# Query and key groups of 512 and 256 tokens instead of 384, with expert scores between them

## The chip, the cores and the metric

The kernel runs on one NeuronCore of a Trainium2 chip. The metric is the device time of one execution in microseconds (us); the median of the runs is compared. The engines are called by the profile's names: PE is TensorE (matmuls; PEld are its weight loads), ACT is ScalarE, DVE is VectorE, POOL is GpSimd, SP issues most of the loads and stores. A "wait" is a semaphore wait: each engine runs its own list of instructions in order and stops where a semaphore is not yet high enough.

## What is computed

Three stages, for 4 sequences of 768 tokens with 384 channels. A gated linear recurrence gives x. A mixture of 4 experts, each a causal attention with 64 channels, takes x; a third stage mixes tokens and channels. The change is in the second stage, which per sequence is:

```python
for e in range(E):                       # 4 experts
    q = x @ wq[e]
    k = x @ wk[e]
    v = x @ wv[e]
    scores = scale * (q @ k.transpose(0, 2, 1))
    scores = np.where(causal, -1000000000.0, scores)
    scores = scores - scores.max(-1, keepdims=True)
    a = np.exp(scores)
    a /= a.sum(-1, keepdims=True) + 1e-09
    ye = a @ v @ wo[e]
    # out += (routing weight of e) * ye
```

## The kernel before

The kernel runs the recurrence and the experts for one sequence after the other (`it` is 0 to 3, called the first to the fourth batch here), then the third stage for all four (from about 324 us on). The recurrence of a batch runs on PE with DVE, ACT and POOL preparing the gates of the next batch in whatever gaps they have. The order on each engine is written out by hand; nothing is planned at run time, and only semaphores tie the engines together.

Within a batch the experts start with "ring" groups: PE writes a group into a PSUM bank, counts `ring_done`; ACT rounds it to a high part, counts `ring_hi`; DVE makes the low part (exact minus rounded), counts `ring_free`. A product of two such split operands is three matmuls (L1253, L1254, L1255: high*high, high*low, low*high). The ring has 6 groups that transpose x (`RING_X`), 6 that make the values and gate logits (260 columns each), then the queries and keys: `qk_h`, `qk_l` with four row blocks m = 0 to 3 of 128 rows, 0 and 1 being the queries of experts 0 and 1, and 2 and 3; blocks 2 and 3 the keys of the same pairs. Before the change each block is made in two halves of 384 tokens, so 8 groups of 9 matmuls (3 chunks of channels, 3 products). Group n writes bank n. `qk_of` gives the order: blocks 0, 2 for the first half, 0, 2 for the second, then blocks 1, 3 twice. `FIRST_JOB = 6` puts the scores of the first job behind the sixth of them.

A "job" m (0 to 5) is a pair of query tiles of 128 tokens, (2,3), (1,4) or (0,5), for one pair of experts: `tiles_of(m)` is `TILES[m // 2]` and the expert pair is `m % 2`. So jobs 0 and 1 look at tiles 2 and 3 and need tokens below 512 only; jobs 2 and 3 need tokens up to 640, jobs 4 and 5 all. Job m has 896 score columns per expert in all: the small tile's columns (`which = 0`) at the end of a two-bank tile, the large tile's (`which = 1`) at its start. Both experts of a job fill all of banks 0 to 3. Per job:

- PE, `expert_scores(m)`: the score matmuls L1399 and the mask L1405, in pieces. It waits (`exp_done`) until ACT has read the previous job's scores: for jobs 1 and 2 the first two exponentials are enough for the first pieces, the last one is needed for the last piece; for jobs 3 to 5 all four are needed before any.
- DVE, `row_max(m)`: four reductions L1121, two for each `which`.
- ACT, `exps(m)`: four exponentials L728, each behind its reduction.
- PE, `turn_probs(m, r)`: 14 transposes of 64 columns (L1316) for expert r = 0 or 1, into a pair of banks given by `turn_pair`: banks 4 and 5, but for (0, 1) banks 6 and 7.
- `copy_turned(m)`: ACT copies r = 0 (L769, counts `pt_copied[1]`), DVE r = 1 (L1141, counts `pt_copied[0]`), about 900 columns each.
- PE, `weigh_values(m)`: 28 matmuls L1462.

PE's order around the change is: groups 0 to 5, scores(0), groups 6 and 7, scores(1) (whose last piece waits for all ring groups), turn(0,0), scores(2) with turn(0,1) in it, turn(1,0), weigh(0), turn(1,1), scores(3), and so on. turn(1,0) goes to the banks of turn(0,0) and so waits for ACT's `copy_turned(0)`. DVE's order is: route (a chain of some 25 small operations, L1091 to L1111), low parts of groups 0 to 5 with a prefix scan (L875, 768 columns) for the next batch behind group 3 in the second and third batch, row_max(0), low parts 6 and 7, row_max(1), the first two reductions of row_max(2), copy_turned(0), the other two of row_max(2), `portions(0)` (three small operations), copy_turned(1), row_max(3). ACT's is: groups 0 to 5, exps(0), groups 6 and 7, exps(1), copy_turned(0), first two of exps(2), copy_turned(1), the other two. In the fourth batch ACT also rounds a tile of the token weights (L621) between group 7 and exps(1).

Of the kernel before, what the change touches and what calls it, by code (L numbers as in the profile page):

```python
# [22 lines left out]
P = 128  # L23
B, H, T, HD = 4, 8, 768, 48
D = H * HD
# [113 lines left out]
def turn_pair(m, r):  # L139

    if m == JOBS - 1:
        return r
    return 3 if (m, r) == (0, 1) else 2
# [47 lines left out]
def build(nc, fT, qT, kT, vT, v, wq, wk, wv, w_gate, wo, woT, w_theta, w_tok, w_ch, out):  # L191
    with ExitStack() as ctx:
# [234 lines left out]
        def _(pool):  # L427
# [64 lines left out]
            def token_weights(tile):  # L492

                s, n = tile // 2, tile % 2
# [34 lines left out]
        def _(act):  # L529
# [87 lines left out]
            def token_weights(tile):  # L617

                s, n = tile // 2, tile % 2
                act.wait_ge(tok_in[s], 16)  # L620
                nc.scalar.copy(wt_h[:, n * NT + s, :], wt_raw[:, n * NT + s, :]).then_inc(tok_hi, 1)  # L621
# [43 lines left out]
            for it in range(B):  # L665
# [64 lines left out]

                for n in [*range(RING_X), *range(FIRST_QK, RING)]:
                    if n == FIRST_QK:
# [17 lines left out]
                    if n == FIRST_QK + FIRST_JOB:  # L750
                        exps(0)
                    act.wait_ge(ring_done, upto(it, RING, n + 1))
                    if n < RING_X:
                        nc.scalar.copy(xT_h[:, :, n * P:(n + 1) * P],
                                       ps(ring_bank(it, n))[:, 0:D].rearrange("p (c t) -> p c t", c=NC)).then_inc(ring_hi, 1)
                    else:
                        half, m = qk_of(n - FIRST_QK)
                        nc.scalar.mul(qk_h[:, m, half * HALF:(half + 1) * HALF], ps(ring_bank(it, n))[:, 0:HALF],
                                                                             ED ** -0.5 if m < 2 else 1.0).then_inc(ring_hi, 1)
                    if n == FIRST_QK + 1 and 1 <= it < B - 1:  # L760
                        grow(it + 1, 2)
                    if it < 1 and n == FIRST_QK + 2:
                        shrink_pair(1, 1)
                    if it < 1 and n == FIRST_QK + 3:
                        grow_pair(1, 1)

# [12 lines left out]
                for j in range(JOBS + 2):  # L779
                    if 1 <= j < JOBS:  # L780
# [76 lines left out]
        def _(dve):  # L857
# [143 lines left out]
            for it in range(B):  # L1001
# [122 lines left out]
                for n in range(RING_QK):  # L1124
                    if n == FIRST_JOB:
                        row_max(0)
                        if it < 1:
                            scan(1, 2)
                    dve.wait_ge(ring_hi, upto(it, SPLIT, RING_X + n + 1))
                    half, m = qk_of(n)  # L1130
                    at = slice(half * HALF, (half + 1) * HALF)
                    nc.vector.scalar_tensor_tensor(out=qk_l[:, m, at], in0=ps(ring_bank(it, FIRST_QK + n))[:, 0:HALF],
                                                   scalar=ED ** -0.5 if m < 2 else 1.0,
                                                   in1=qk_h[:, m, at].bitcast(F32), op0=ALU.mult,
                                                   op1=ALU.subtract).then_inc(ring_free, 1)
                    if 1 <= it < B - 1 and n == 3:
                        scan(it + 1, 3)
# [31 lines left out]
                for j in range(JOBS + 2):  # L1169
                    if 1 <= j < JOBS:  # L1170
# [79 lines left out]
        def _(pe):  # L1250
# [61 lines left out]
            for it in range(B):  # L1312
# [69 lines left out]
                def expert_scores(m):  # L1382

                    a = m % 2
                    if m < 1:
                        pe.wait_ge(ring_free, upto(it, RING, FIRST_QK + 4))
                        pe.wait_ge(halves, 128)
                    elif m == 1:
                        pe.wait_ge(ring_free, upto(it, RING, FIRST_QK + 6))
# [25 lines left out]
                    if m == 1:  # L1415
                        pe.wait_ge(ring_free, upto(it, RING, RING))
# [6 lines left out]
                def turn_probs(m, r):  # L1423
# [43 lines left out]
                for n in range(RING):  # L1467
# [9 lines left out]
                    if n == FIRST_QK + FIRST_JOB:  # L1477
                        expert_scores(0)
                    if n < 4:
                        pe.wait_ge(a_masked, upto(it, NT, NT))  # L1480
                    elif n < FIRST_QK and it < B - 1:
# [5 lines left out]
                    elif n < FIRST_QK + 4:  # L1487
                        pe.wait_ge(ring_free, upto(it, RING, n - 3))
                    elif it > B - 2 and n == FIRST_QK + 4:
                        banks_read(0, EARLY)  # L1490
# [7 lines left out]
                    elif n >= FIRST_QK:  # L1498
                        half, m = qk_of(n - FIRST_QK)
                        if n == FIRST_QK:  # L1500
                            pe.wait_ge(wqk_lo, 1)
                        for c in range(NC):
# [134 lines left out]
```

## Time and profile before

| | |
|---|---|
| median of 3 runs | 568.0 us (567.95 to 569.58) |
| the profiled execution's own time | 570.03 us |
| its span, first to last instruction | 568.3 us |
| PE matmuls busy | 538.7 us, 95% of the span |
| DVE, ACT, POOL busy | 371.8, 298.1, 132.0 us (65%, 52%, 23%) |
| TensorE clock granted | 1.000 over the whole span (2.4 GHz) |
| query and key groups start, four batches | 53.91, 127.12, 199.98, 277.37 us |

A busy share of PE counts from the start of a matmul to its modelled end; matmuls overlap, so what a stretch costs is read from start to start. A time written as "+17.65" below is counted from the start of the batch's first query and key group.

### The profile page before, as it was taken

The page shows a single profiled execution, that of the slowest core. Times are in us where ns is not written, and L with a number is a line of the kernel's source. Part 1 is how long each engine was busy: PE and PEld are TensorE (multiplying, and loading weights), DVE is VectorE, ACT ScalarE, POOL GpSimd, SP SyncE. Part 2 cuts the span into 40 slices and gives each one's busy share as a digit, 9 for nine tenths or more (in the row PEclk, how much of TensorE's full clock was granted, in tenths as well). Part 3 has the DMA queues.
Part 4 walks back from the last instruction along what each step waited for, and adds up shares of the span by engine and source line. Part 5 has one row for each costly group of instructions (what it writes and reads, how often), then busy time and mean ns, then how long its engine had stood idle before and what let it go on. Part 6 is the DMA issues. An engine that isn't in the chain of part 4 may idle for free.

```text
span 568.3 us, 14108 instructions
## 1 busy us (share of the span) xinstructions
PE 538.7 (95%) x5996; PEld 508.8 (90%) x5996; DVE 371.8 (65%) x672; ACT 298.1 (52%) x599; POOL 132.0 (23%) x88
## 2 busy tenths in 40 slices
PE   0989999999999999999999999999999999999997
PEld 0688878999789997899978899999999999999997
DVE  2988888878788787775768677555236544462434
ACT  5758687775877548733568664324222433133311
POOL 2003046035510025200022357112211212022200
PEclk9999999999999999999999999999999999999999
DMA  8948013052210430003600000010001100020002
GB/s 289 321 151 301 7 27 86 7 196 112 76 39 3 159 151 2 2 2 104 233 1 2 1 1 2 0 57 29 0 1 43 42 1 1 14 71 1 1 1 83
DMA packets 17969, 37.24 MB, mean 66 GB/s; under 512 B 2160, under 2 KB 10608, under 8 KB 17392
## 3 DMA queue, kind: packets, MB, share of 16 engines
q1 hardware_dynamic: 17904, 36.32, 18.5%
q8 instruction: 47, 0.77, 0.6%
q14 instruction: 18, 0.15, 0.1%
HBM read 31.46 MB, written 4.72 MB: 64 GB/s over the span
## 4 chain that ended last, share of the span: by engine, by line
PE 79%; DVE 8%; ACT 7%; issue 3%; DMA 2%; SPq 1%; DVEq 0%; ACTq 0%
PE bank L1253 18%; PE bank L1254 18%; PE bank L1255 17%; ACT prob L728 5%; PE bank L1462 4%; PE bank L1271 4%; PE bank L1399 4%; PE bank L1316 3%; PE bank L1358 3%; PE bank L1354 2%; DMA OT<-w_theta 2%; PE bank L1339 2%; PE bank L1562 1%; DVE gate L875 1%; DVE nmax L1121 1%
## 5 line engine op out<-in xcount | busy, mean ns | idle before, releaser
L1253 PE MATMUL bank<-z_h,wt_h 128*128 128x384 f32 x288 | 97.7, 339 | 0.0
L1254 PE MATMUL bank<-z_l,wt_h 128*128 128x384 f32 x288 | 97.4, 338 | 0.0
L1255 PE MATMUL bank<-z_h,wt_l 128*128 128x384 f32 x288 | 96.5, 335 | 0.0
L728 ACT ACTIVATE prob<-bank,nmax 128x384 f32<-128x384 f32 (+5 forms) x96 | 60.3, 638 | 20.7 <-DVE nmax L1121 20.7
L524 POOL TENSOR_TENSOR trig<-trig,x 128x768 f32<-128x768 f32 x18 | 33.6, 1865 | 149.6 <-ACT trig L634 92.6
L1121 DVE TENSOR_REDUCE nmax<-bank 128x1 f32<-128x384 f32 (+5 forms) x96 | 54.9, 616 | 10.0 <-PE bank L1405 5.3
L967 DVE TENSOR_SCALAR turns<-bank 128x384 int32<-128x384 f32 x22 | 12.2, 556 | 74.1 <-PE bank L1255 74.1
L1253 PEld LDWEIGHTS bank<-z_h,wt_h 128*128 128x128 f32 x288 | 54.0, 188 | 0.6 <-issue 0.3
L1254 PEld LDWEIGHTS bank<-z_l,wt_h 128*128 128x128 f32 x288 | 54.1, 188 | 0.0
L1255 PEld LDWEIGHTS bank<-z_h,wt_l 128*128 128x128 f32 x288 | 54.0, 188 | 0.0
L843 ACT CAST uT_h<-bank 128x384 fp32r<-128x384 f32 x24 | 11.5, 479 | 78.6 <-PE bank L1562 78.6
L1462 PE MATMUL bank<-probT,Vm 128*64 128x128 f32 x672 | 42.0, 276 | 0.7 <-DVE probT L1141 0.2
L1462 PEld LDWEIGHTS bank<-probT,Vm 128*64 128x64 f32 x672 | 36.2, 137 | 2.9 <-DVE probT L1141 1.4
L626 ACT COPY x<-bank 128x384 f32<-128x384 f32 x24 | 11.6, 481 | 49.8 <-PE bank L1255 44.5
L1007 DVE TENSOR_TENSOR probT<-bank,keep 128x1024 f32<-128x1024 f32 x24 | 29.3, 1221 | 12.0 <-PE bank L1271 11.9
L1358 PE MATMUL bank<-V,probT 128*64 128x48 f32 x768 | 36.1, 219 | 0.4 <-DVE probT L1007 0.3
L1399 PE MATMUL bank<-qk_h 64*128 64x512 f32 (+3 forms) x128 | 26.2, 406 | 7.1 <-ACT prob L728 5.4
L1358 PEld LDWEIGHTS bank<-V,probT 128*64 128x64 f32 x768 | 32.2, 137 | 0.8 <-issue 0.6
L1253 PE MATMUL bank<-xT_h,wqk_h 128*128 128x384 f32 x96 | 32.9, 343 | 0.0
L1254 PE MATMUL bank<-xT_l,wqk_h 128*128 128x384 f32 x96 | 32.4, 337 | 0.0
L1255 PE MATMUL bank<-xT_h,wqk_l 128*128 128x384 f32 x96 | 32.4, 337 | 0.0
L1354 PE MATMUL bank<-S,q 128*64 128x96 f32 x320 | 28.8, 255 | 2.6 <-DVE S L1028 1.9
(177 smaller groups left out, 1398.5 us busy)
## 6 DMA issues: line engine op xcount, KB each, us to landing
V<-v SPq DMA_DIRECT2D x4, 1152.0 KB, 11.1
gate<-fT SPq DMA_DIRECT2D x12, 384.0 KB, 3.2
q<-qT SPq DMA_DIRECT2D x12, 384.0 KB, 6.2
k<-kT SPq DMA_DIRECT2D x12, 384.0 KB, 6.5
wt_raw<-w_tok SPq DMA_DIRECT2D x6, 768.0 KB, 8.5
out<-x SPq DMA_DIRECT2D x24, 192.0 KB, 1.9
gate<-fT SPq DMA_DIRECT2D x3, 512.0 KB, 5.1
q<-qT SPq DMA_DIRECT2D x3, 512.0 KB, 9.5
```

The costliest lines, as they stand in the source:

```text
L524: nc.gpsimd.tensor_tensor(trig[:, s % 2, :, :], trig[:, s % 2, :, :], x2[:, s:s + 1, :].broadcast_to([P, 2, D]), ALU.mult).then_inc(z_made, 1)
L728: nc.scalar.activation(prob[:, m % 2, r, at], bank[r][:, at], ACT.Exp, bias=nmax[:, m, k:k + 1], accum_out=den[:, m // 2, which, e:e + 1]) ...
L1007: nc.vector.tensor_tensor(Am[:, c % 2, :, :], bank[c % 2][:, :].rearrange("p (h t) -> p h t", h=H), keep[:, None, :].broadcast_to([P, H, P ...
L1121: nc.vector.tensor_reduce(nmax[:, m, k:k + 1], bank[r][:, columns_of(m, which)], X, ALU.max, negate=True).then_inc(max_done, 1)
L1253: nc.tensor.matmul(o, a_h, b_h, start=start, stop=False)
L1254: nc.tensor.matmul(o, a_h, b_l, start=False, stop=False)
L1255: return nc.tensor.matmul(o, a_l, b_h, start=False, stop=stop)
L1271: mm = nc.tensor.matmul(bank[c % 2][:, slot(h):slot(h) + P], k[r:r + 64, h // 2, at], q[r:r + 64, h // 2, at], start=True, stop=True)
L1354: nc.tensor.matmul(ps(out_bank(c))[own, h * HD:(h + 2) * HD], q[:, h // 2, c * P + own.start:c * P + own.stop], S[:, c % 2, h // 2, :], st ...
L1358: mm = nc.tensor.matmul(ps(out_bank(c))[own, h * HD:(h + 1) * HD], Am[:, c % 2, slot(h) // P, own], V[:, c, h * HD:(h + 1) * HD], start=(c ...
L1399: mm = nc.tensor.matmul(bank[r][:, lo_:hi_], x[rows, a, queries], y[rows, 2 + a, keys], start=fresh_bank and n == 0, stop=False, skip_grou ...
L1462: mm = nc.tensor.matmul(ps(values_bank(m))[64 * r:64 * r + 64, at], Vm[:, s, e * ED:(e + 1) * ED], probT[:, m % 2, r, n * P:(n + 1) * P], ...
```

## The change

The queries and keys are made in 7 groups: blocks 0, 2, 1, 3 for tokens 0 to 511 (512 columns each), then blocks 0 and 2 for tokens 512 to 767 (256 columns each), then one group with blocks 1 and 3 for tokens 512 to 767 (two of 256 columns in one bank). Groups 0 to 3 come ahead of scores(0), 4 and 5 between scores(0) and scores(1), and the seventh (`LATE_QK = 6`) behind scores(2) and turn(1,0). The number of matmuls and of their columns stays the same, and so does the number of columns on ACT and DVE; the banks, the waits and the orders on DVE and ACT change as the diff shows. In the fourth batch the token weights of a tile pair are taken in the other order.

```diff
-RING_X, RING_QK, RING_V = NT, 8, NT
+RING_X, RING_QK, RING_V = NT, 7, NT
-FIRST_JOB = 6
+FRONT = 4 * P
+LATE_QK = 6
 def qk_of(n):
-    return n % 4 // 2, (0, 2, 1, 3)[2 * (n // 4) + n % 2]
+    if n < 4:
+        return [((0, 2, 1, 3)[n], slice(0, FRONT), slice(0, FRONT))]
+    if n < LATE_QK:
+        return [((0, 2)[n - 4], slice(FRONT, T), slice(0, T - FRONT))]
+    return [(1, slice(FRONT, T), slice(0, T - FRONT)), (3, slice(FRONT, T), slice(T - FRONT, 2 * (T - FRONT)))]
 def ring_bank(it, n):
     if n >= FIRST_QK:
-        return n - FIRST_QK
+        return (0, 1, 6, 7, 4, 5, 6)[n - FIRST_QK]
 def turn_pair(m, r):
-    return 3 if (m, r) == (0, 1) else 2
+    return 3 if (m, r) == (0, 0) else 2
 # POOL and ACT, token_weights
-                s, n = tile // 2, tile % 2
+                s, n = tile // 2, 1 - tile % 2
 # ACT
-                for n in [*range(RING_X), *range(FIRST_QK, RING)]:
+                for n in range(RING_X): ...            # x as before
+                for n in range(LATE_QK):
...
-                    if n == FIRST_QK + FIRST_JOB:
+                    if n == 4:
                         exps(0)
+                    split_qk(n)
...
+                exps(1)
                 for j in range(JOBS + 2):
-                    if 1 <= j < JOBS:
+                    if 2 <= j < JOBS:
                         exps(j, range(0, 2))
-                    if 2 <= j <= JOBS:
+                    if 1 <= j <= JOBS:
                         copy_turned(j - 1)
-                    if 1 <= j < JOBS:
-                        exps(j, range(2, EXPS))
-                    if j == 1:
-                        copy_turned(0)
+                    if 2 <= j < JOBS:
+                        exps(j, range(2, 3))
+                    if j == 2:
+                        split_qk(LATE_QK)
+                    if 2 <= j < JOBS:
+                        exps(j, range(3, EXPS))
 # DVE
+                split_qk(0)
+                split_qk(1)
+                if 1 <= it < B - 1:
+                    scan(it + 1, 3)
+                split_qk(2)
+                if it < 1:
+                    scan(1, 2, 0)
+                split_qk(3)
+                row_max(0)
+                if it < 1:
+                    scan(1, 2, 1)
+                split_qk(4)
+                row_max(1, range(0, 2))
+                split_qk(5)
+                row_max(1, range(2, EXPS))
...
-                    if it < 1 and j == 1:
+                    if it < 1 and j == 2:
                         scan(1, 3, 0)
-                    if j == 1:
-                        row_max(2, range(0, 2))
+                    if j == 2:
+                        split_qk(LATE_QK)
                     if 1 <= j <= JOBS:
                         copy_turned(j - 1)
+                    if j == 1:
+                        row_max(2, range(0, 2))
 # PE, expert_scores
-                    if m < 1:
-                        pe.wait_ge(ring_free, upto(it, RING, FIRST_QK + 4))
+                    if m < 3:
+                        pe.wait_ge(ring_free, upto(it, RING, FIRST_QK + 2 * m + 2))
                         pe.wait_ge(halves, 128)
-                    elif m == 1:
-                        pe.wait_ge(ring_free, upto(it, RING, FIRST_QK + 6))
+                    elif m == 3:
+                        pe.wait_ge(ring_free, upto(it, RING, RING))
...
-                    if m == 1:
-                        pe.wait_ge(ring_free, upto(it, RING, RING))
 # PE, turn_probs
-                    elif m == 1:
-                        pe.wait_ge(pt_copied[1], upto(it, JOBS, 1))
-                    elif m >= 2:
+                    elif m >= 1:
                         pe.wait_ge(pt_copied[0], upto(it, JOBS, m))
 # PE
+                def queries_keys(n):
+                    if n < 2:
+                        pe.wait_ge(ring_free, upto(it, RING, FIRST_V + 2 + n + 1))
+                    elif it > B - 2 and n == 2:
+                        banks_read(0, EARLY)
+                    elif n == LATE_QK:
+                        pe.wait_ge(pt_copied[1], upto(it, JOBS, 1))
...
+                for n in range(4):
+                    queries_keys(n)
+                expert_scores(0)
+                queries_keys(4)
+                queries_keys(5)
+                expert_scores(1)
                 for j in range(1, JOBS + 2):
-                    if j < JOBS:
+                    if 2 <= j < JOBS:
                         expert_scores(j)
...
+                    if j == 2:
+                        queries_keys(LATE_QK)
                     if j >= 2:
                         weigh_values(j - 2)
```

## Rows read from the trace of the kernel before

**Rows 1.** Waits of PE: engine line <- who ended it: us in total, times, longest.

```profile
PE bank L1399 <- ACT prob L728: 5.4, 15, 0.7
```

**Rows 2.** Timeline of PE, third batch: start us, us, engine, line, operation, form, idle before.

```profile
198.03 0.28 PE L1255 MATMUL bank<-wvg_h,xT_l 128*128 128x260 f32 x1
199.98 0.34 PE L1253 MATMUL bank<-xT_h,wqk_h 128*128 128x384 f32 x1
...
209.58 0.44 PE L1399 MATMUL bank<-qk_h 64*128 64x384 f32 x2
...
211.31 0.44 PE L1253 MATMUL bank<-xT_h,wqk_h 128*128 128x384 f32 x1
...
214.66 0.44 PE L1399 MATMUL bank<-qk_h 64*128 64x384 f32 x2
...
217.63 0.39 PE L1399 MATMUL bank<-qk_h 64*128 64x256 f32 x2 [0.20 <-ACT prob L728]
...
218.69 0.60 PE L1316 MATMUL bank<-ident,prob 64*128 64x64 f32 x14
219.26 0.49 PE L1399 MATMUL bank<-qk_h 64*128 64x512 f32 x2
...
220.06 0.65 PE L1316 MATMUL bank<-ident,prob 64*128 64x64 f32 x14
...
223.34 0.39 PE L1399 MATMUL bank<-qk_h 64*128 64x256 f32 x2 [0.30 <-ACT prob L728]
```

**Rows 3.** Timeline of ACT, third batch, the exponentials of jobs 0 and 1.

```profile
211.27 0.58 ACT L728 ACTIVATE prob<-bank,nmax 128x384 f32<-128x384 f32 x1 [1.09 <-DVE nmax L1121]
...
213.72 0.50 ACT L758 ACTIVATE qk_h<-bank 128x384 fp32r<-128x384 f32 x1
...
216.91 0.57 ACT L728 ACTIVATE prob<-bank,nmax 128x384 f32<-128x384 f32 x1
...
218.44 0.68 ACT L728 ACTIVATE prob<-bank,nmax 128x512 f32<-128x512 f32 x1
...
219.10 0.91 ACT L769 COPY probT<-bank 128x896 f32<-128x896 f32 x1
```

**Rows 4.** Timeline of DVE, third batch, low parts, row maxima and the first copy.

```profile
210.21 0.56 DVE L1132 SCALAR_TENSOR_TENSOR qk_l<-bank,qk_h 128x384 fp32r<-128x384 f32 x1 [0.50 <-ACT qk_h L758]
210.69 2.21 DVE L1121 TENSOR_REDUCE nmax<-bank 128x1 f32<-128x384 f32 x4
...
215.76 1.01 DVE L1121 TENSOR_REDUCE nmax<-bank 128x1 f32<-128x384 f32 x2
...
218.90 0.76 DVE L1121 TENSOR_REDUCE nmax<-bank 128x1 f32<-128x256 f32 x2 [0.57 <-PE bank L1405]
219.57 1.08 DVE L1141 COPY probT<-bank 128x896 f32<-128x896 f32 x1
```

**Rows 5.** Timeline of DVE and PE, second batch.

```profile
134.16 1.95 DVE L1132 SCALAR_TENSOR_TENSOR qk_l<-bank,qk_h 128x384 fp32r<-128x384 f32 x4
136.03 1.74 DVE L875 TENSOR_TENSOR_SCAN gate<-fresh,gate 128x768 f32<-128x768 f32 x1
...
138.60 1.00 DVE L1121 TENSOR_REDUCE nmax<-bank 128x1 f32<-128x384 f32 x2
...
127.12 0.34 PE L1253 MATMUL bank<-xT_h,wqk_h 128*128 128x384 f32 x1
...
150.69 0.39 PE L1399 MATMUL bank<-qk_h 64*128 64x256 f32 x2 [0.32 <-ACT prob L728]
```

**Rows 6.** Timeline of PE, first and fourth batch: first group and start of scores(3).

```profile
53.91 0.34 PE L1253 MATMUL bank<-xT_h,wqk_h 128*128 128x384 f32 x1
...
77.28 0.38 PE L1399 MATMUL bank<-qk_h 64*128 64x256 f32 x2
...
277.37 0.34 PE L1253 MATMUL bank<-xT_h,wqk_h 128*128 128x384 f32 x1
...
300.72 0.39 PE L1399 MATMUL bank<-qk_h 64*128 64x256 f32 x2 [0.32 <-ACT prob L728]
```

More of the change, by code:

```diff
@@ L617, in token_weights @@
             def token_weights(tile):
-                s, n = tile // 2, tile % 2
+                s, n = tile // 2, 1 - tile % 2
                 act.wait_ge(tok_in[s], 16)
@@ L729, in exps, with split_qk @@
                                              accum_out=den[:, m // 2, which, e:e + 1]).then_inc(exp_done, 1)
-                for n in [*range(RING_X), *range(FIRST_QK, RING)]:
-                    if n == FIRST_QK:
+                def split_qk(n):
+                    act.wait_ge(ring_done, upto(it, RING, FIRST_QK + n + 1))
+                    for m, tokens, at in qk_of(n):
+                        ins = nc.scalar.mul(qk_h[:, m, tokens], ps(ring_bank(it, FIRST_QK + n))[:, at],
+                                            ED ** -0.5 if m < 2 else 1.0)
+                    ins.then_inc(ring_hi, 1)
+                for n in range(RING_X):
+                    act.wait_ge(ring_done, upto(it, RING, n + 1))
+                    nc.scalar.copy(xT_h[:, :, n * P:(n + 1) * P],
+                                   ps(ring_bank(it, n))[:, 0:D].rearrange("p (c t) -> p c t", c=NC)).then_inc(ring_hi, 1)
+                for n in range(LATE_QK):
+                    if n < 1:
                         if it > B - 2:
@@ L1122, in row_max, with split_qk @@
                                                 negate=True).then_inc(max_done, 1)
[L1124 to L1128, printed above, removed]
-                    dve.wait_ge(ring_hi, upto(it, SPLIT, RING_X + n + 1))
[L1130 to L1137, printed above, removed]
+                def split_qk(n):
+                    dve.wait_ge(ring_hi, upto(it, SPLIT, RING_X + n + 1))
+                    for m, tokens, at in qk_of(n):
+                        ins = nc.vector.scalar_tensor_tensor(out=qk_l[:, m, tokens], in0=ps(ring_bank(it, FIRST_QK + n))[:, at],
+                                                             scalar=ED ** -0.5 if m < 2 else 1.0,
+                                                             in1=qk_h[:, m, tokens].bitcast(F32), op0=ALU.mult,
+                                                             op1=ALU.subtract)
+                    ins.then_inc(ring_free, 1)
+                split_qk(0)
[13 more added lines that the diff above has]
+                row_max(1, range(2, EXPS))
                 def copy_turned(m):
@@ L1169, in _ @@
                 for j in range(JOBS + 2):
-                    if 1 <= j < JOBS:
+                    if 2 <= j < JOBS:
                         row_max(j, range(2 if j == 2 else 0, EXPS))
@@ L1465, in weigh_values @@
                     mm.then_inc(av_done, 1)
-                for n in range(RING):
+                def queries_keys(n):
[5 more added lines that the diff above has]
+                        pe.wait_ge(pt_copied[1], upto(it, JOBS, 1))
+                    if n < 1:
+                        pe.wait_ge(wqk_lo, 1)
+                    for m, tokens, at in qk_of(n):
+                        w = slice(m * P, (m + 1) * P)
+                        for c in range(NC):
+                            mm = split_mm(ps(ring_bank(it, FIRST_QK + n))[:, at], wqk_h[:, c, w], wqk_l[:, c, w],
+                                          xT_h[:, c, tokens], xT_l[:, c, tokens], c == 0, c == NC - 1)
+                    mm.then_inc(ring_done, 1)
+                for n in range(FIRST_QK):
                     if it > B - 2 and n == 0:
@@ L1497, in _ @@
                             mm = nc.tensor.transpose(dst[:, c * P:(c + 1) * P], xn[:, n, c * P:(c + 1) * P], ident[:, :])
[L1498 to L1502, printed above, removed]
-                            at = slice(half * HALF, (half + 1) * HALF)
-                            w = slice(m * P, (m + 1) * P)
-                            mm = split_mm(dst[:, 0:HALF], wqk_h[:, c, w], wqk_l[:, c, w], xT_h[:, c, at],
-                                          xT_l[:, c, at], c == 0, c == NC - 1)
                     else:
```

23 lines of the change are left out of this document (6 added, 17 removed).

## The prediction

> **What bounds the kernel now.** I read the page first (PE 95% busy, full clock), then who PE waits for, then the timelines of PE, ACT and DVE from the first query and key group to the fourth job's scores. All waits of the scores on ACT's exponentials are 5.4 us in 15 places [rows 1]: a mean of 0.36 us. So PE is nearly the bound, and right behind it stands a loop through three engines: scores, row maxima on DVE, exponentials on ACT, next scores. scores(3) starts the moment the last exponential of job 2 is read, after 0.30 us idle, though PE had its other work done [rows 2]. From there on each job hangs on that loop, and it starts from scores(3). So I measure the change by one number: how late scores(3) starts after the batch's first group. Before it is +23.36 in the third batch [rows 2], +23.57 in the second [rows 5], +23.37 and +23.35 in the first and fourth [rows 6]. What moves scores(3) moves the rest of the batch.
>
> **What does not change.** Matmuls of 260 columns go at (199.98 - 198.03)/16 = 0.122 us, of 384 at (209.58 - 199.98 - 0.10)/54 = 0.176, the 0.10 being the switch to another kind [rows 2]. That is 0.436 ns a column, so I take 0.232 for 512 and 0.120 for 256. No row has 512 columns on 128 rows; by proportion it would be 0.235 and not less than the 0.176 of 384. Old: 72 x 0.176 = 12.67 us. New: 36 x 0.232 + 36 x 0.120 = 12.67. Nothing is saved on PE. ACT and DVE have the same columns and eight split operations each as before. The change is one of order.
>
> A rule of the Trainium skill, "TensorE: Matmul & The Clock Gate", section "Back-to-back issue gap", gives N/2.4 + 2.5 ns: 0.216 for 512, 0.1625 for 384, 0.109 for 256. By it the old six groups would take 8.78 us and the new four 7.77, 1.01 earlier instead of the 1.15 below, so 0.14 us a batch worse than my sum. The trace's 384-column gap is 0.176, so it does not agree, and the sum goes by the rows.
>
> **Third batch, step by step** (times from the first group):
> - Groups 0 to 3 end at 36 x 0.232 = +8.35; scores(0) starts at +8.45, before at +9.60 [rows 2].
> - But DVE makes the low part of group 3 ahead of row_max(0). The group is whole at +8.54 (its last matmul 0.23 before the end, and some 0.4 to drain). The split of 384 columns takes ACT 0.50 and DVE 0.56, the next operation starting 0.48 on [rows 3, 4]. No row has 512 columns: the bounds are those values and 4/3 of them; I take 0.60 on ACT and 0.60 to DVE's next. Row_max(0) starts at 8.54 + 0.60 + 0.04 + 0.60 = +9.8, before +10.71 [rows 4]. The exponentials follow 0.58 later (211.27 - 210.69) and take 2.45 in all (to 213.72) [rows 3]: +10.4 to +12.8.
> - PE: scores(0) takes 1.73, groups 4 and 5 18 x 0.120 = 2.16 and 0.18 for switches (211.31 to 214.66 was 18 x 0.176 + 0.18) [rows 2]. scores(1) starts at 8.45 + 1.73 + 2.34 = +12.5, before +14.68. Its last piece needs the last exponential of job 0, read at +13.0, just in time. It ends at +14.2, turn(0,0) at +14.75.
> - ACT splits groups 4 and 5 only behind exps(0): from +12.8, each 0.39 (bounds 0.33 and 0.50). DVE, idle since +12, makes the low part of 4 at +13.25 (0.34 to the next, bounds 0.32 and 0.48), then two maxima of job 1 at +13.6 and +14.1, low part 5 at +14.55, the other two at +14.9. First two exponentials of job 1 at +14.2 and +14.75; PE may go on 0.72 after the start of the second (216.91 to 217.63) [rows 2, 3]. So scores(2) starts at **+15.5**, before +17.65: 2.2 earlier, but PE has put off 2.3 us of work and has been idle 0.7.
> - turn(0,1) starts 1.06 behind scores(2), +16.5. The last piece of scores(2) needs job 1's last exponential: it starts at +16.3, 0.82 later (218.44 to 219.26) PE goes: +17.1, and 0.80 later is through, +17.9 [rows 2, 3].
> - The new wait: turn(1,0) now goes to the banks of turn(0,1), which DVE copies. DVE can start 0.69 behind the turn, +17.2, and needs 1.08 [rows 4] and 0.05 to be seen: turn(1,0) at +18.35, 0.44 late. Row_max(2) is queued behind that copy, at +18.2: before it ran ahead of the copy, 1.27 behind the scores (218.90) [rows 2, 4], now 2.7 behind.
> - From turn(1,0) to scores(3) were 3.28 us, 0.30 of them idle [rows 2]; with the last group's 18 x 0.120 + 0.10 that is 2.98 + 2.26 = 5.24. The exponentials of job 2 with the late split among them are read at about +22.9, so they hide. scores(3) starts at 18.35 + 5.24 = **+23.6**: 0.22 later than before.
>
> The POOL and SP queues are passed by nothing: no DMA or POOL operation moves but the order of the fourth batch's token tiles, whose first use is far behind. There ACT's rounding of a tile comes behind exps(1), +16.9 to +17.7, and copy_turned(0) ends at +18.6, still ahead of exps(2) at +18.7. So first and fourth batch are as the third: 23.58 against 23.37 and 23.35 [rows 6], +0.21 and +0.23.
>
> **Second batch.** Here DVE comes to the low parts only at +7.04 (134.16 - 127.12) [rows 5]. Two of 512 columns, the scan (1.66 to the next), two more: 7.04 + 4 x 0.60 + 1.66 = +11.1 for row_max(0), before +11.48 (138.60) [rows 5]. The old order hid this behind groups 6 and 7. Now exponentials run +11.7 to +14.1; scores(1) waits for two until +13.0 and its last piece until +14.3; the low parts 4 and 5 and job 1's maxima follow, its second exponential starts at +16.05, scores(2) at +16.8, turn(0,1) +17.8, DVE's copy +18.5, turn(1,0) +19.65, scores(3) at **+24.9**, against +23.57 [rows 5]: +1.3.
>
> **Sum:** 0.21 + 1.3 + 0.22 + 0.23 = +2.0 us. The profiled execution, 568.3 of span in 570.03, would be 572.0; on the median of 568.0 it is **570.0**. The unknown widths move the chain by 0.4 either way a batch (four operations of 0.1): 568.4 to 571.6 for this case.
>
> A second page speaks against wide groups: "Perfetto Trace Analysis", section "Optimizing Scalar/DVE Operations", says that where these engines are not saturated but hold others up, broken-up operations may let work end sooner. Here DVE is busy 65%, and the wide group costs the first maxima 0.10 + 0.12 us against a 384-column one, by the estimates above; no row shows the wide one.
>
> **Rivals.**
> - *The late second batch does not bind.* If DVE's lateness is taken up, say because the first maxima come between, all batches lose 0.22: +0.9, 568.9, no change to be measured. For it: three of four batches look like that. Against: DVE's queue in the second is full from the routing on [rows 5].
> - *Faster: the put-off group fills PE's idle time.* Without any wait the new order costs PE 8.45 + 1.73 + 2.34 + 1.65 + 0.57 (turn) + 1.06 + 0.57 + 0.80 + 5.24 = +22.4 to scores(3), 0.95 under the old +23.36: 564.2 for four batches. The place is scores(2) and turn(1,0), with 0.7 and 0.44 of wait by my sum; faster needs the two together under half. For it: the first maxima do come 0.9 earlier. Against: the chain of two splits and two maxima behind exps(0) is in order on two engines.
> - *Slower: DVE's copy ahead of row_max(2) and the late split on ACT make job 2's last exponential the bound in each batch.* It has 0.6 us of room; if the low parts or the turn come 1.7 later, as in the second batch's lateness, each batch loses about 1.3: +5.3, 573.3.
>
> **Chances.** My sum 0.52, hidden 0.23, faster 0.13, all batches late 0.12. Measurement tells apart about 0.3%, 1.7 us. Of my sum's range 568.4 to 571.6 about a third lies under 569.7: 0.17 of same. So faster 0.13, same 0.17 + 0.23 = 0.40, slower 0.35 + 0.12 = 0.47. The range from 566.5 (a small part of the faster case) to 573.0 leaves out some 0.15. The likeliest case alone is 568.4 to 571.6.
>
> **What would show it.** scores(0) at +8.45 and scores(2) at +15.5 in the third batch; an idle of 0.4 before turn(1,0) ended by DVE's probT copy; scores(3) at +23.6, in the second batch at +24.9 with idle ahead of scores(1). Groups of 512 at 0.232 a matmul. The job loop behind scores(3) as long as before, 5.2 us. I am wrong if the waits ahead of scores(2) or turn(1,0) are missing, if scores(3) is earlier than +23.4, or if a later stage takes the loss up.

## The result and the profile after

The changed kernel takes 570.32 us in the median of 16 runs (569.15 to 571.77), the kernel before beside it 569.32 (567.95 to 571.26): a ratio of 1.0024, 95% interval 1.0013 to 1.0035, which is 1.4 us more; the two medians themselves are 1.0 apart. The forecast was 2.0 more. The profiled execution took 570.51, its span 568.8. All ratios in this document leave out executions far above the others, of which there was one: 1319.38 us, the fourth of e5.

The page says little; PE is as busy as before, DVE and ACT too:

```profile
span 568.8 us, 14113 instructions
...
PE 536.6 (94%) x5996; PEld 502.1 (88%) x5996; DVE 371.8 (65%) x673; ACT 298.0 (52%) x599; POOL 132.5 (23%) x88
```

The waits of PE (engine, line <- who ended it: us in total, times, longest) show what is new, a wait of each turn(1,0) on DVE's copy, once a batch, and 8.2 us on exponentials where [rows 1] had 5.4:

```profile
PE bank L1427 <- ACT prob L737: 8.2, 14, 1.0
...
PE bank L1344 <- DVE probT L1167: 1.4, 4, 0.4
```

A wait that the kernel before had in scores(1), on low parts, is gone:

```profile
PE bank L1399 <- DVE qk_l L1132: 1.5, 4, 0.5
```

The loss can't be had by adding these up, since idle time is counted from the modelled end of a matmul; it is read from start to start below.

PE's timeline in the third batch (start, us, engine, line, operation, form, idle before), against [rows 2]:

```profile
200.36 0.40 PE L1281 MATMUL bank<-xT_h,wqk_h 128*128 128x512 f32 x1
...
208.82 0.45 PE L1427 MATMUL bank<-qk_h 64*128 64x384 f32 x2
...
212.88 0.45 PE L1427 MATMUL bank<-qk_h 64*128 64x384 f32 x2
...
215.93 0.39 PE L1427 MATMUL bank<-qk_h 64*128 64x256 f32 x2 [0.81 <-ACT prob L737]
...
218.76 0.65 PE L1344 MATMUL bank<-ident,prob 64*128 64x64 f32 x14 [0.36 <-DVE probT L1167]
...
223.35 0.65 PE L1344 MATMUL bank<-ident,prob 64*128 64x64 f32 x14
223.81 0.36 PE L1427 MATMUL bank<-qk_h 64*128 64x256 f32 x2
```

scores(0), (1) and (2) start at +8.46, +12.52 and +15.57: 1.1, 2.2 and 2.1 ahead of the kernel before. turn(1,0) comes at +18.40 and scores(3) at +23.45, and there nothing is left of the lead: before it was +23.36. Ahead of scores(3) stands no idle any more: it starts 0.46 behind turn(1,1), the 14 transposes at 223.35. In the kernel before it started 0.96 behind them (223.34 in [rows 2]):

```profile
222.38 0.65 PE L1316 MATMUL bank<-ident,prob 64*128 64x64 f32 x14
```

ACT in that batch, against [rows 3], and DVE, against [rows 4]:

```profile
208.92 0.60 ACT L743 ACTIVATE qk_h<-bank 128x512 fp32r<-128x512 f32 x1 [1.50 <-PE bank L1283]
...
210.75 0.58 ACT L737 ACTIVATE prob<-bank,nmax 128x384 f32<-128x384 f32 x1 [1.22 <-DVE nmax L1137]
```

```profile
209.56 0.69 DVE L1143 SCALAR_TENSOR_TENSOR qk_l<-bank,qk_h 128x512 fp32r<-128x512 f32 x1 [1.10 <-ACT qk_h L743]
210.16 2.21 DVE L1137 TENSOR_REDUCE nmax<-bank 128x1 f32<-128x384 f32 x4
...
217.61 1.09 DVE L1167 COPY probT<-bank 128x896 f32<-128x896 f32 x1 [1.11 <-PE bank L1344]
218.62 0.74 DVE L1137 TENSOR_REDUCE nmax<-bank 128x1 f32<-128x256 f32 x2
```

The second batch is the one that loses more. Its PE and DVE, against [rows 5]:

```profile
126.36 0.40 PE L1281 MATMUL bank<-xT_h,wqk_h 128*128 128x512 f32 x1
...
139.45 0.44 PE L1427 MATMUL bank<-qk_h 64*128 64x384 f32 x2 [0.49 <-ACT prob L737]
...
143.25 0.39 PE L1427 MATMUL bank<-qk_h 64*128 64x256 f32 x2 [1.02 <-ACT prob L737]
...
146.09 0.65 PE L1344 MATMUL bank<-ident,prob 64*128 64x64 f32 x14 [0.36 <-DVE probT L1167]
...
151.14 0.36 PE L1427 MATMUL bank<-qk_h 64*128 64x256 f32 x2
```

```profile
133.44 1.29 DVE L1143 SCALAR_TENSOR_TENSOR qk_l<-bank,qk_h 128x512 fp32r<-128x512 f32 x2
134.65 1.75 DVE L891 TENSOR_TENSOR_SCAN gate<-fresh,gate 128x768 f32<-128x768 f32 x1
136.31 1.26 DVE L1143 SCALAR_TENSOR_TENSOR qk_l<-bank,qk_h 128x512 fp32r<-128x512 f32 x2
137.49 2.20 DVE L1137 TENSOR_REDUCE nmax<-bank 128x1 f32<-128x384 f32 x4
```

DVE works without a gap from +7.1 to +13.3 and is the last to come to row_max(0), at +11.1. In the first batch DVE has two halves of a scan more than in the others ahead of row_max(3), one ahead of the late low part (to 75.56) and one behind its copy of turn(1,1):

```profile
75.56 0.73 DVE L1143 SCALAR_TENSOR_TENSOR qk_l<-bank,qk_h 128x256 fp32r<-128x256 f32 x2
76.49 1.09 DVE L1167 COPY probT<-bank 128x896 f32<-128x896 f32 x1 [0.20 <-PE bank L1344]
77.50 0.95 DVE L891 TENSOR_TENSOR_SCAN gate<-fresh,gate 128x384 f32<-128x384 f32 x1
78.36 0.73 DVE L1137 TENSOR_REDUCE nmax<-bank 128x1 f32<-128x256 f32 x2
```

The late low part ends at 76.29, +23.48, and scores(3) starts at +23.53.

Counted in each batch from its first group to the end of its last weigh_values (the fourth: the start of it), and for scores(3):

| batch | scores(3) before | after | end of the experts before | after | lost |
|---|---|---|---|---|---|
| first | +23.38 | +23.53 | +45.56 | +45.96 | 0.40 |
| second | +23.56 | +24.78 | +45.23 | +46.42 | 1.19 |
| third | +23.36 | +23.45 | +45.02 | +45.09 | 0.07 |
| fourth | +23.35 | +23.44 | +44.99 | +45.06 | 0.07 |

Together 1.73 us. From the first batch's first group to the end of the span the traces have 514.41 before and 515.99 after, 1.58 more. (The first group itself starts between 51.5 and 53.9 in the profiled executions of this study, so a span alone says less than this difference.)

### The profile page after: what moved, and what is told of

It reads as the page before. It is cut to its first block, busy times and chain, and to the rows that moved or that the text cites. A ratio compares the mean times of both kernels' runs of the same rounds, so it can differ in the third digit from the quotient of the medians.

```text
span 568.8 us, 14113 instructions
## 1 busy us (share of the span) xinstructions
PE 536.6 (94%) x5996; PEld 502.1 (88%) x5996; DVE 371.8 (65%) x673; ACT 298.0 (52%) x599; POOL 132.5 (23%) x88
## 4 chain that ended last, share of the span: by engine, by line
PE 78%; DVE 9%; ACT 8%; issue 3%; DMA 1%; SPq 0%; DVEq 0%; ACTq 0%
PE bank L1281 18%; PE bank L1282 17%; PE bank L1283 17%; PE bank L1486 6%; ACT prob L737 5%; PE bank L1344 4%; PE bank L1299 4%; PE bank L1427 3%; PE bank L1386 3%; DVE probT L1167 2%; PE bank L1382 2%; PE bank L1367 1%; PE bank L1597 1%; DVE gate L891 1%; DMA gate<-fT 1%
## 5 line engine op out<-in xcount | busy, mean ns | idle before, releaser
L1167 DVE COPY probT<-bank 128x896 f32<-128x896 f32 x24 | 26.1, 1088 | 14.7 <-PE bank L1344 14.7
L1281 PE MATMUL bank<-xT_h,wqk_h 128*128 128x512 f32 (+1 forms) x96 | 33.3, 347 | 0.0
L1282 PE MATMUL bank<-xT_l,wqk_h 128*128 128x512 f32 (+1 forms) x96 | 32.5, 338 | 0.0
L1283 PE MATMUL bank<-xT_h,wqk_l 128*128 128x512 f32 (+1 forms) x96 | 32.4, 338 | 0.0
```

The lines of the kernel that those rows point to most:

```text
L1167: nc.vector.tensor_copy(probT[:, m % 2, 1, :].rearrange("p (c h q) -> p h c q", h=2, q=64), turned(m, 1)).then_inc(pt_copied[0], 1)
L1281: nc.tensor.matmul(o, a_h, b_h, start=start, stop=False)
L1282: nc.tensor.matmul(o, a_h, b_l, start=False, stop=False)
L1283: return nc.tensor.matmul(o, a_l, b_h, start=False, stop=stop)
```

## The experiments

All ratios are to the kernel before, on the same chip. Where four start times of scores(3) are given, they are those of the four batches, each from the start of the batch's first group. Start times are from one profiled execution of each kernel. "..." in a diff stands for lines left out.

**e1_scan_in_halves.** The changed kernel, with the prefix scan for the next batch taken out from between the low parts in the second and third batch and put behind the maxima in two halves.

```diff
-                if 1 <= it < B - 1:
-                    scan(it + 1, 3)
...
                 row_max(0)
                 if it < 1:
                     scan(1, 2, 1)
+                elif it < B - 1:
+                    scan(it + 1, 3, 0)
...
                 row_max(1, range(2, EXPS))
+                if 1 <= it < B - 1:
+                    scan(it + 1, 3, 1)
```

> The changed kernel, with the scan of the second and third batch taken from between the low parts 1 and 2 on DVE and run in two halves, one behind row_max(0), one behind row_max(1). Theory A (DVE's lateness in the second batch makes most of the loss): there row_max(0) starts at +9.8 instead of +11.1, scores(1) at +12.5 without idle, scores(3) at +23.5 instead of +24.8; the other batches keep +23.45; the time falls by 1.1 to 1.3 us, ratio to the kernel before 1.000 (0.999 to 1.001). Theory B (the loss is spread over all batches or comes from elsewhere, and the second batch only waits in another place): scores(3) of the second batch stays at +24.4 or later and the ratio at 1.002.

Measured: 1.0087 (1.0065 to 1.0109), slower, where the two theories had 1.000 and 1.002: neither foresaw this. The first part did what it should: in the second batch scores(1) is at +12.53, scores(2) at +15.57 and turn(1,0) at +18.42, as in the third. But scores(3) is at +25.55, in the third batch at +25.59. DVE of the second batch:

```profile
141.38 0.94 DVE L891 TENSOR_TENSOR_SCAN gate<-fresh,gate 128x384 f32<-128x384 f32 x1
...
146.18 1.67 DVE L1176 TENSOR_SCALAR share<-den 128x8 f32<-128x8 f32 x1
147.88 0.20 DVE L1178 RECIPROCAL share<-share 128x8 f32<-128x8 f32 x1
148.12 2.03 DVE L1180 TENSOR_TENSOR spread<-share,wroute 128x512 f32<-128x512 f32 x1
150.07 0.74 DVE L1143 SCALAR_TENSOR_TENSOR qk_l<-bank,qk_h 128x256 fp32r<-128x256 f32 x2
```

`portions(0)`, 0.16 and 0.69 us elsewhere, takes 1.67 and 2.03, and the late group's low part is queued behind it. POOL meanwhile:

```profile
142.41 1.84 POOL L473 TENSOR_TENSOR q<-q,decay 128x768 f32<-128x768 f32 x1 [13.40 <-DVE gate L891]
...
145.99 1.83 POOL L473 TENSOR_TENSOR q<-q,kTs 128x768 f32<-128x768 f32 x1
147.78 1.81 POOL L476 TENSOR_TENSOR k<-k,gate 128x768 f32<-128x768 f32 x1
```

The first ends with the POOL instruction that runs beside it (147.85 and 147.82). The second, 0.69 elsewhere, ends 0.56 behind the next one of POOL (150.15 and 149.59), as if it had worked only from there on. POOL scales the next batch's queries and keys once the last scan is done; a later scan put that work on top of `portions(0)`. So DVE's lateness does cause the early loss, but the place I gave the scan costs more. Part of the 1.0087 is a lower clock behind the new wait, told at the end.

**e2_banks_swapped.** The changed kernel; the turned probabilities go to the banks of before, so that turn(1,0) waits for ACT's copy and the late group for DVE's.

```diff
-        return (0, 1, 6, 7, 4, 5, 6)[n - FIRST_QK]
+        return (0, 1, 4, 5, 6, 7, 6)[n - FIRST_QK]
...
-    return 3 if (m, r) == (0, 0) else 2
+    return 3 if (m, r) == (0, 1) else 2
...
-                    elif m >= 1:
+                    elif m == 1:
+                        pe.wait_ge(pt_copied[1], upto(it, JOBS, 1))
+                    elif m >= 2:
...
                     elif n == LATE_QK:
-                        pe.wait_ge(pt_copied[1], upto(it, JOBS, 1))
+                        pe.wait_ge(pt_copied[0], upto(it, JOBS, 1))
```

> The changed kernel, with groups 2 to 5 in banks 4, 5, 6, 7 and the turns in the banks of the kernel before, so that turn(1,0) waits for ACT's copy and the seventh group for DVE's. Theory A (turn(1,0) stands 0.5 us behind DVE's copy of turn(0,1) in each batch): turn(1,0) starts at +17.9 instead of +18.4, scores(3) at +23.0 in first, third and fourth batch, +24.3 in the second; four times -0.4 to -0.45, -1.7 us, ratio 0.9995. Theory B (the wait only moves: the seventh group then waits for DVE's copy and job 2's exponentials end too late): scores(3) stays at +23.4, ratio 1.002.

Measured: 0.9996 (0.998 to 1.0012). Against the changed kernel about 0.28% is won, 1.6 us; from the first batch's first group to the end of the span the trace has 514.97, 1.0 less than the changed kernel. In the third batch, whose first group starts at 199.557:

```profile
217.45 0.65 PE L1344 MATMUL bank<-ident,prob 64*128 64x64 f32 x14
...
222.49 0.36 PE L1427 MATMUL bank<-qk_h 64*128 64x256 f32 x2
```

turn(1,0) at +17.89 with no idle, scores(3) at +22.93, 0.52 earlier; in the second batch +24.21, 0.57 earlier. The first and fourth stay at +23.54 and +23.66, each held by something else: the first by the low part of the late group, which stands behind half a scan on DVE (PE idle 0.43 ahead of scores(3)), the fourth by ACT's copy, behind the rounding of a token tile (0.57 ahead of turn(1,0)). So the wait on DVE's copy binds, and there is more behind it in two batches.

**e3_seventh_ahead.** The deferral undone: the seventh group stands ahead of scores(1), its splits behind those of 4 and 5. The diff leaves out the lines taken away at its old places.

```diff
+                split_qk(LATE_QK)                # ACT
                 exps(1)
...
-                row_max(1, range(0, 2))          # DVE
                 split_qk(5)
-                row_max(1, range(2, EXPS))
+                split_qk(LATE_QK)
+                row_max(1)
...
                 queries_keys(5)                  # PE
+                queries_keys(LATE_QK)
                 expert_scores(1)
```

> The changed kernel, with the seventh group not put off: groups 4, 5 and 6 all between scores(0) and scores(1), their splits behind exps(0) and ahead of exps(1). Theory A (the early start of job 1 pays back nearly all that the put-off group costs, so putting it off is about neutral and undoing it makes things worse): scores(1) at +14.7, scores(2) at +18.0, scores(3) at +23.8 in the third batch, +0.45 against before; ratio 1.003 to 1.004. Theory B (the put-off group in the middle of job 2 is itself the loss): scores(3) comes back to +23.36, ratio 1.000.

Measured: 1.0088 (1.0067 to 1.0109), slower than I had expected (1.003 to 1.004, scores(3) at +23.8): scores(3) is at +24.65 to +24.67 in all four batches. PE in the third, first group at 203.282:

```profile
221.36 0.39 PE L1422 MATMUL bank<-qk_h 64*128 64x256 f32 x2 [0.30 <-ACT prob L737]
...
224.19 0.65 PE L1341 MATMUL bank<-ident,prob 64*128 64x64 f32 x14 [0.34 <-DVE probT L1166]
...
227.93 0.39 PE L1422 MATMUL bank<-qk_h 64*128 64x256 f32 x2 [0.83 <-ACT prob L737]
```

The wait ahead of scores(2) shrinks from 0.81 to 0.30, but the one on DVE's copy stays and 0.83 comes up ahead of scores(3). The maxima of job 2 stand behind DVE's copy (224.06 behind 223.05), and with no late group between turn(1,0) and scores(3) nothing hides them. The deferral is a gain inside the change, not its cost.

**e4_both_edits** (e1 and e2 together).

> Scan in halves and swapped banks together. Theory A (two separate waits, one in the second batch, one in all): the gains add, scores(3) at +23.0 in all four batches, 0.4 under the kernel before in each, -1.5 us, ratio 0.997. Theory B (both edits open the same slack, or the exponentials of job 2 bind next): no better than the better one of the two, ratio 0.9995 or more.

Measured: 1.0093 (1.0068 to 1.0118), where 0.997 was expected if the gains add: scores(3) at +23.53, +25.55, +25.57, +23.66. In the middle batches it is e1's loss, in the last e2's token tile. POOL's meeting with `portions(0)` covers all that the banks give in the middle batches. This run could not test whether the gains add; e8 does.

**e5_pool_held** (e1, and POOL's scaling waits for `portions(0)`).

```diff
-                    elif p == PAIRS // 2:
+                    elif b > 1 and p == 0:
                         pool.wait_ge(spread_done, upto(b - 1, len(TILES), 1))
```

> The kernel with the scan in halves (1.0087), with one thing changed on POOL alone: in the second and third batch its scaling of q and k for the next batch waits for portions(0) of this batch on DVE. Theory C (in that kernel the scan ended later, so POOL's four operations of 1.84 us ran back to back into DVE's small operations of portions(0), which stood still until each POOL operation was over, 1.67 and 2.03 us instead of 0.16 and 0.69; the late low part behind them held scores(3) by 2 us): portions(0) takes 1.1 us again, scores(3) is at +23.5 in the second and third batch instead of +25.6, and with the second batch now free of its late start the ratio is 1.000 (0.999 to 1.002). Theory D (DVE's own order is at fault, POOL only stands beside it): portions(0) stays slow or something else holds the late low part, scores(3) at +25 or later, ratio over 1.005.

Measured: `portions(0)` is back at its short times, scores(3) at +23.45 in the second and third batch. DVE and POOL, second batch:

```profile
146.50 0.16 DVE L1176 TENSOR_SCALAR share<-den 128x8 f32<-128x8 f32 x1
146.93 0.69 DVE L1180 TENSOR_TENSOR spread<-share,wroute 128x512 f32<-128x512 f32 x1
...
158.51 1.80 DVE L1176 TENSOR_SCALAR share<-den 128x8 f32<-128x8 f32 x1
160.59 2.03 DVE L1180 TENSOR_TENSOR spread<-share,wroute 128x512 f32<-128x512 f32 x1
```

```profile
158.47 1.81 POOL L473 TENSOR_TENSOR q<-q,OT 128x768 f32<-128x768 f32 x1
```

That settles what took e1's time. But POOL's eight instructions, starting later, now run into `portions(1)` (1.80 and 2.03), PE waits 1.1 for it in each of the two batches, and the experts end at +47.3: 1.0100 (1.0066 to 1.0134) over three executions, where 1.000 was expected. The loss moved by one job pair.

**e6_scan_as_first.** The changed kernel; the scan in halves of which the first stays among the low parts and the second stands directly behind row_max(0), the order that the first batch has.

```diff
-                if 1 <= it < B - 1:
-                    scan(it + 1, 3)
                 split_qk(2)
-                if it < 1:
-                    scan(1, 2, 0)
+                if it < B - 1:
+                    scan(it + 1, 2 if it < 1 else 3, 0)
                 split_qk(3)
                 row_max(0)
-                if it < 1:
-                    scan(1, 2, 1)
+                if it < B - 1:
+                    scan(it + 1, 2 if it < 1 else 3, 1)
```

> The changed kernel, with the scan of the second and third batch in halves as the first batch has it: one between low parts 2 and 3, one behind row_max(0). Theory A with C (the second batch loses by DVE's lateness, and POOL must have started early enough not to meet portions(0)): the scan ends at about +13.2, POOL's four operations at about +20.5, just ahead of portions(0) at +20.8; in the second batch row_max(0) at +10.3, scores(2) at +16.1, scores(3) at +23.9 to +24.0 instead of +24.8, third batch unchanged at +23.45; ratio 1.001. Theory B (second batch's loss is not DVE's lateness): scores(3) stays at +24.8.

Measured: 1.0011 (0.9999 to 1.0024). scores(3) in the second batch at +23.95 instead of +24.78, the others unchanged; the experts of the second batch end at +45.59, 0.83 earlier. By the traces the four batches lose 0.90 us to the kernel before instead of 1.73, by the ratio 0.6. All start times came as expected. The ratio alone doesn't tell this kernel from the changed one (1.0013 to 1.0035), and the medians are 1.0 above the kernel before in both; that 0.83 is won is the traces' word.

**e7_banks_and_ends** (e2; the first batch's scan half behind the late low part, the fourth's token tile behind ACT's first copy).

```diff
-                        if j < 1:
+                        if j == 1:
                             token_weights(0)
...
+                    if j == 2:
+                        split_qk(LATE_QK)
                     if it < 1 and j == 2:
                         scan(1, 3, 0)
-                    if j == 2:
-                        split_qk(LATE_QK)
```

> The kernel with swapped banks (0.9996), with two orders mended: in the first batch the half scan on DVE comes behind the late low part, in the fourth ACT's rounding of a token tile behind its first copy. Expected if these two named orders were what kept the first and fourth batch from gaining: scores(3) at +22.95 to +23.05 in the first (was +23.54) and +22.95 in the fourth (was +23.66), second and third as they were (+24.2, +22.9); 0.5 to 1.0 us less, ratio 0.998. If something else holds them (POOL, job 2's exponentials), they stay at +23.5 and the ratio at 0.9996.

Measured: 1.0003 (0.9989 to 1.0017), where 0.998 was expected. scores(3) at +22.92, +24.22, +22.93, +22.92: the two batches that e2 left are freed. It is not to be told from e2 by the ratio (their intervals overlap); the traces show it. In the first batch the gain is given back by the next operation: scores(4) at +29.13, where scores(3) is 0.6 earlier, since the second half of the scan stands ahead of row_max(3).

**e8_banks_ends_scan** (e7 and e6).

> All three: swapped banks, the two orders, and the scan as in the first batch. If the waits are separate, the gains add: scores(3) at +23.0, +23.4, +22.9 and +22.95, 1.4 us in all under the kernel before, ratio 0.9975. If portions(0), which comes 0.4 us earlier here, now meets POOL in the second or third batch, scores(3) there is at +24.5 or later and the ratio at 1.001 or more.

Measured: 0.9993 (0.9977 to 1.001), where 0.9975 was expected. scores(3) at +22.92, +23.41, +22.93, +22.92: the edits add up in the traces, with 0.97 us less than before over four batches; the ratio doesn't tell it from no change.

**e9_all_and_first_scan** (e8, and the first batch's last scan one place earlier in both halves: behind row_max(1) and behind the late low part).

```diff
                 row_max(1, range(2, EXPS))
+                if it < 1:
+                    scan(1, 3, 0)
...
                     if it < 1 and j == 2:
-                        scan(1, 3, 0)
+                        scan(1, 3, 1)
...
-                    if it < 1 and j == 2:
-                        scan(1, 3, 1)
```

> The kernel with swapped banks, mended orders and divided scan (0.9993), with the first batch's scan of pair 3 moved: its first half behind row_max(1), where DVE stands idle from +16.1 to +17.2, its second half behind the late low part. If the scan in front of row_max(3) is what gave the first batch's gain back (scores(4) at +29.14, before +29.03), scores(4) comes at +28.1 and the batch's end 1.0 us earlier; 2.0 us in all under the kernel before, ratio 0.9965 (0.995 to 0.998). If POOL, which starts when that scan is done, then meets a two-input operation of DVE that the loop waits for, the first batch's scores(4) or (5) come later than before and the ratio is over 1.000.

Measured: 0.9965 (0.995 to 0.998), 566.96 us beside 568.83. It beats both kernels. In its list of waits none of turn(1,0) is left:

```profile
PE bank L1425 <- ACT prob L737: 6.9, 12, 1.0
```

The first batch's scores(4) is at +28.30 (+28.1 expected), and its experts end at +44.84, 0.72 ahead of before; over the four batches 0.72 + 0.11 + 0.44 + 0.45 = 1.72 us less, 2.0 by the ratio.

**e10_changed_again** (the changed kernel as it is, on the chip of e9).

> The changed kernel once more, unedited, beside the version above on the same chip: ratio 1.002 to 1.003 as before, and the version above faster than it by 3 us.

Measured: 1.0022 (1.0008 to 1.0037), 570.65 beside 568.83. The result repeats, and e9's gain, 3.7 us against this run, is not the chip's.

## Why the prediction was right, step by step

- *Nothing saved on PE.* 36 matmuls of 512 columns went from 200.36 to 208.72 (0.10 for the switch): 0.232 each, as predicted. scores(0) came at +8.46, +8.45 predicted.
- *The widths no row had.* 512 columns took ACT 0.60 and DVE 0.60 to its next operation, the values taken. Row_max(0) at +9.80, as worked out.
- *Third batch.* scores(1) +12.52 (12.5), scores(2) +15.57 (15.5) with 0.81 idle (0.7), turn(1,0) +18.40 (18.35) with 0.36 idle ended by DVE's copy (0.44), row_max(2) behind that copy at +18.26 (18.2).
- *The term that was mis-sized: 5.24 us from turn(1,0) to scores(3).* Measured 5.05. I took the old stretch less the 0.30 that its row shows as idle and added the late group. But idle is counted from the modelled end of the last transpose, 0.65 behind its row's start, and where nothing waits scores(3) starts 0.46 behind that row (223.35 to 223.81). So the old wait (222.38 to 223.34, 0.96) was 0.50 long and not 0.30: 0.20 too much in my sum. The rest nearly cancels: the late group took 2.34 with its switch (2.26 taken), and turn(1,0) 0.58 to the next operation (0.64 before). So scores(3) is at +23.45 instead of +23.6, in the second to fourth batch 0.12 to 0.15 less than predicted (first 0.05), and the loss in the third and fourth 0.07 instead of 0.22.
- *Second batch.* Row_max(0) +11.1 (11.1), scores(1) +13.09 (13.0), scores(2) +16.90 (16.8), turn(1,0) +19.73 (19.65), scores(3) +24.78 (24.9). The loss is 1.19, predicted 1.3. e6 shows the cause: with half of the scan away from the low parts 0.83 of it goes. The loop behind scores(3) is as long as before, as predicted: 5.20 to scores(4) in the third batch, 5.22 before.
- *First batch.* 0.40 instead of 0.21. I had not looked at where `scan(1, 3, ...)` goes. Its first half now stands ahead of the late low part and holds scores(3): +0.15, where the third and fourth batch lose 0.09. Its second half stood ahead of row_max(3) in the kernel before too; but through it row_max(3) follows DVE's copy of turn(1,1), which starts 0.39 later than before (+23.68 and +23.29), and not scores(3) as in the other batches. e9 moves both halves, and scores(4) comes 1.1 earlier than in the changed kernel, 0.84 earlier than in e8.
- *What was luck.* The sum of 2.0 is near the 1.7 of the traces because two errors cancel in part: the third and fourth batch lose 0.31 less than predicted, the first 0.19 more. And the time, 570.0 against 570.32, is nearer than the loss, 2.0 against 1.4, since the kernel before came out at 569.32 and not at the 568.0 that I started from.
- *Rival "the put-off group fills PE's idle time".* It needs the waits ahead of scores(2) and turn(1,0) together under half; they are 1.17 (0.81 + 0.36). It did not come. But e2 shows how near it is: without the 0.36, scores(3) is at +22.93, ahead of the +23.36 of before. In that batch the bank pair decides the sign; over all four e2 still loses 0.56 us to the kernel before by the traces, since the second batch and the ends stay.
- *Rival "late second batch does not bind".* Refuted: 1.2 of the 1.7 us are there.
- *Rival "job 2's last exponential binds in each batch".* Not in the changed kernel, where scores(3) has no idle ahead of it. In e3, without the group between, it does bind, with 0.83.

What is shown: the two causes, DVE's late first maxima in the second batch (e6) and DVE's copy ahead of turn(1,0) in each (e2, e7), and that they add up (e8, e9). They are shown by start times, of one profiled execution of each kernel; of the mended kernels only e9 is apart from the kernel before in time. What stays open: what it would be worth to move POOL's work that makes DVE late in the second batch, and when exactly the clock falls (both below).

## What to carry to other kernels

In a hand-ordered kernel in which a producer's lead is traded for later work, follow one start time (here scores(3)) through each batch, each engine's queue included; two batches lost 0.07 each, the first, with a scan at another place, 0.40, and the second, with a fuller DVE queue, 1.19. When a reordering frees a start but gives it back, look for the bank or buffer whose reader changed engine: exchanging two banks moved scores(3) of the third batch by 0.52 us, the whole change by 0.09. And moving a small operation "to where the engine is idle" is only free if nothing waits for it: POOL waited for the scan.

## What the runs showed of the hardware

**DVE stands still beside POOL.** A `TENSOR_SCALAR` on 128x8 took 0.16 us alone and 1.67 to 1.80 beside POOL's 1.8-us instructions, `spread` 0.69 alone and 2.03; a `RECIPROCAL` (0.20) and the low parts, which read PSUM (0.74), kept their time. The stand-still is inside the duration of the DVE instruction and not in its idle time, so it is found by comparing one form at different places. The same is part of why DVE is late in the second batch, in both kernels: L1108's 24-column product took 1.62 us where it takes 0.18 in the other three batches, beside 4.13 us of POOL, and the scan ahead of it 2.69 instead of 1.75 (in the kernel before 1.61 and 2.68). In the changed kernel:

```profile
124.88 2.69 DVE L891 TENSOR_TENSOR_SCAN gate<-fresh,gate 128x768 f32<-128x768 f32 x1
...
128.47 1.62 DVE L1108 TENSOR_TENSOR rt<-Vm,rt 128x24 f32<-128x24 f32 x1
```

```profile
121.64 4.32 POOL L479 TENSOR_TENSOR wx_l<-OT,wx_h 128x768 fp32r<-128x768 f32 x2 [18.65 <-ACT wx_h L605]
125.92 4.13 POOL L479 TENSOR_TENSOR wch_l<-OT,wch_h 128x1152 fp32r<-128x1152 f32 x1
```

L1108's product ends at 130.09 and POOL's instruction at 130.05. No run moved POOL's work here, so what it costs the batch is not shown. The Trainium skill, "SBUF — State Buffer", section "Who interferes with whom", says that DVE and POOL share a port pair as an exclusive lock: a DVE instruction with two SBUF inputs contends with a POOL instruction that reads SBUF, in a mode that uses both ports whoever comes second blocks for the whole instruction of the other, and a DVE instruction with at most one SBUF input outside those modes does not contend. By that rule the trace agrees for the two-input product, the scan, `spread` and the unaffected low parts and `RECIPROCAL`; for the small `TENSOR_SCALAR` it agrees only if that ran in such a mode, which no row shows.

**The clock after a short wait.** In e1 PE waited 1.89 us for the late low part in the second batch, after a stretch with less work, and the granted clock was under 1.00 in the stretches that follow (stretch in us, its length, busy time of PE, PEld, DVE, ACT, POOL, granted clock, DMA share, GB/s):

```profile
125.30:148.00 22.70, 21.52 (x206) 17.67 (x206) 20.98 (x49) 14.36 (x38) 9.30 (x5) 1.00 0.26 94
148.00:153.00 5.00, 3.11 (x48) 2.57 (x45) 4.53 (x7) 1.38 (x5) 4.37 (x3) 0.89 0.40 125
153.00:160.00 7.00, 7.00 (x116) 6.18 (x114) 3.76 (x8) 5.29 (x17) 4.03 (x3) 0.84 0.21 59
```

Means of 0.89 and 0.84 are part of the stretch at 1.2 GHz and the rest at 2.4. The like wait of e1's third batch, 1.94 us, left 1.00. In e4 PE waited 2.44 and 2.46 in these places, and the clock fell behind both; its third batch has, where e1 has 1.00:

```profile
225.00:230.00 5.00, 3.08 (x26) 2.81 (x27) 3.62 (x6) 0.45 (x2) 4.37 (x4) 0.69 0.00 0
```

The price: from scores(3) to scores(4) it took 6.40 us (e1, second batch), 6.30 and 6.75 (e4), against 5.21 at 1.00 (e1, third batch), 1.1 to 1.5 us more. It is not one execution alone: the mean granted clock was 0.997 in four of six executions of e1, 0.994 to 0.997 in five of six of e4 and 0.997 in two of the three of e5, against one of 17 of the kernel before on the chip of e1, two of 12 of e2, and none under 0.999 in the 28 of the changed kernel (with e10). So it is a second price that a moved wait can have, and the ratios of e1, e4 and e5 hold it.
